# One loop over the steps of all tiles and both layers, with x split a tile ahead

## The chip, the core and the metric

The kernel runs on one core of a Trainium2 chip. The metric is the device time of one execution in microseconds (us); a lower time is better. Engines are named as in the profile: PE (TensorE), PEld (its weight loads), DVE (VectorE), ACT (ScalarE), POOL (GpSimd), SP (SyncE, which issues the transfers here).

## The reference

Attention without a softmax over keys, then two feed-forward layers on the same 2304 tokens of width 512:

```python
batch, n_heads, seq, head_dim = (4, 8, 576, 64)
# attention, per batch and head
q_s = exp(q - max(q, axis=-1));  q_s = q_s / (sum(q_s, axis=-1) + 1e-09)
k_s = exp(k - max(k, axis=2));   k_s = k_s / (sum(k_s, axis=2) + 1e-09)
kv = einsum('bhsd,bhse->bhde', k_s, v)
x = einsum('bhsd,bhde->bhse', q_s, kv)      # reshaped to (2304, 512)
# layer 1
h = x @ w_in                                 # (2304, 2048)
r = maximum(h, 0.0);  g = s * (r * r) + b
x = g @ w_out                                # (2304, 512)
# layer 2, other weights
h = x @ w_in
sp = log1p(exp(minimum(h, 20.0)))            # h itself where h > 20
g = h * tanh(sp)
out = g @ w_out
```

## The kernel before

Every fp32 product is made of three matmuls: each operand is split into a high part (a rounded copy, made by ACT) and a low part (the rest, made by DVE), and the products high*high, high*low and low*high are summed in one PSUM bank.

The tokens are cut into five tiles: tiles 0 to 3 have 512 tokens (`TILE`), tile 4 (`FULL`) has 256 (`LAST`). Layer 1 takes them in the order 0 to 4, layer 2 in the order 0, 4, 1, 2, 3 (`B_ORDER`). A tile has 16 steps (`FC`), one for each 128 columns of the 2048. A step of a tile is, on PE, `up` (12 matmuls into one of the H banks) and `down_a` or `down_b` (12 matmuls into the four Y banks, which sum over all 16 steps of a tile). `up` of a step runs `LAG_A` = 3 steps ahead of `down_a` in layer 1, and `LAG_B` = 4 steps ahead of `down_b` in layer 2, because ACT and DVE work on the step in between:

- layer 1: ACT `relu`, DVE `square`, ACT `g_hi`, DVE `g_lo`. `relu` of a step also waits until the slot of g that it writes has been used, that is for `down_a` of three steps before, which PE runs directly after the `up` of the same step. `up` uses two H banks (`HA`), and waits for the `relu` of two steps before.
- layer 2: ACT `exp_h`, DVE `min_e` and `m_of_e`, ACT twice in `rough_inverse`, DVE `rough_ratio`, `unity`, `ratio`, `gate`, ACT `g_hi_b`, DVE `g_lo_b`. DVE works on three steps at once. `up` uses four H banks (`HB`), and waits for the `gate` of four steps before.

Each tile ends with a drain: PE runs the last three or four `down` with no `up` between them. Meanwhile ACT and DVE split the next tile's x into `xs_hi` and `xs_lo` (`split_hi`, `split_lo`; the pair has one buffer, so the split waits for the last `up` of the tile), and then copy Y out of PSUM (`take_y`: banks 0 and 2 by ACT, 1 and 3 by DVE). Then the next tile begins with three or four `up` and no `down`.

The attention for the next batch is cut into four units (two heads each), which run inside the steps of layer 1 in the tiles 0 to 2, a unit every four steps: in the step that a unit starts DVE does `q_max`, `q_shift`, `k_max`, and at the end `q_sum`, `q_eps`, `q_inv`, `q_scale`; one step on `k_shift` (DVE) and `k_exp` (ACT); three steps on PE does `q_transpose` and `kv_product`, and DVE `kv_norm`; five steps on PE does `x_product` and DVE `take_x`. ACT copies the transposes out of PSUM (`take_qT`), and `kv_product`, which writes to the same bank, waits for that copy (`qT_taken`). The q of a unit is loaded when the q of the unit before has been transposed, its k and v when `kv_product` of the unit before is done. The weights are split inside the steps too: in tile 0 by the tables `FIRST_HI` (ACT) and `FIRST_LO` (DVE), in tile 4 by `NEXT_HI` and `NEXT_LO`, in the first tile of layer 2 by `LATE_PARTS`.

All engines work through their own instructions in the order of the program; only semaphores tie them together. Middle tiles are written once in a loop (`Fori`), the others in line.

Of the kernel before, what the change touches and what calls it, by code (L numbers as in the profile page):

```python
# [12 lines left out]
P = 128  # L13
# [9 lines left out]
def linear_attention_moe_kernel(nc, q, k, v, w_in1, w_out1, s, b, w_in2, w_out2, out):  # L23
# [27 lines left out]
    with ExitStack() as ctx:  # L51
# [153 lines left out]
        @block.sync
        def _(sp):
# [61 lines left out]
            with sp.Fori(0, NEXTRA - 1) as t:  # L268
                for p in range(1, NP):
                    load_unit(Unit(t + 1, p))  # L270
                load_unit(Unit(t + 2, 0))
            for p in range(1, NP):
                load_unit(Unit(NEXTRA, p))
# [55 lines left out]
        def _(act):  # L329
# [30 lines left out]
            def split_hi(T, src, x_units=None, parts=range(KC)):  # L360
                w = width(src)
                if not isinstance(T, int) or T > 0:
                    act.wait_ge(h_ready, FC * T)
                for i in parts:
                    if x_units is not None:
                        act.wait_ge(x_taken, 2 * (x_units + i + 1))
                    nc.scalar.activation(xs_hi[:, i, 0:w], xy_tile(i, src, w), ACT.Copy).then_inc(xhi_done, 1)

            def relu(T, f, w):
                c = FC * T + f  # L370
                act.wait_ge(h_ready, c + 1)
                if f >= LAG_A:
                    act.wait_ge(g_used, (FC - 1) * T + f - LAG_A + 1)
                nc.scalar.activation(g_raw[:, f % LAG_A, 1, 0:w], Hb[f % HA][:, 0:w], ACT.Relu).then_inc(ha_taken, 1)  # L374

            def g_hi(T, f, w):
                act.wait_ge(sq_done, FC * T + f + 1)
                nc.scalar.activation(g[:, f % LAG_A, 0, 0:w], g_raw[:, f % LAG_A, 1, 0:w], ACT.Identity,  # L378
                                     bias=b_col[:]).then_inc(ghi_done, 1)

            def take_y(T, src, w, banks, rows=False):
                for i in range(0, banks, 2):
                    act.wait_ge(y_ready, T + i + 1)
                    dst, y = (xy_tile(i, src, w), Y[i][:, 0:w]) if not rows else (
                        last_rows(i), Y[i].rearrange("p (a n) -> p a n", n=LAST))
                    nc.scalar.activation(dst, y, ACT.Copy).then_inc(y_taken_act, 1)
# [521 lines left out]
```

## Time and profile before

| | |
|---|---|
| median of 3 runs | 901.88 us (899.53 to 903.38) |
| the profiled execution's own time | 902.98 us |
| its span, first to last instruction | 901.2 us |
| mean granted TensorE clock | 0.981 of full speed; 0.50 from 503.0 to 506.4 and from 629.3 to 636.1 us |
| PE / DVE / ACT busy | 95% / 68% / 42% of the span |
| layer 2 begins | 488.2 us |
| bytes read and written | 36.15 MB, mean 40 GB/s |

"Busy" counts the time in which an engine executes; the ends of matmuls are modelled. A wait is idle time of an engine before an instruction, put down to the instruction whose end released it. Below, distances between the starts of neighbouring instructions are used where they run back to back, since that is what each costs its engine.

### The profile page before, as it was taken

What the parts mean: (1) busy time and instruction counts of PE and PEld (TensorE: products, weight loads), DVE (VectorE), ACT (ScalarE), POOL (GpSimd) and SP (SyncE); (2) the same over time, 40 slices, a digit from 0 to 9 for tenths busy, and PEclk for the clock granted to TensorE, in tenths of its full rate; (3) what the DMA queues carried; (4) which work ended last, traced back from release to release, by engine and by line L of the source; (5) the groups of instructions that cost most, each with busy time, mean ns of one, the idle gap of its engine ahead of it and who ended that gap; (6) DMA issues with size and microseconds to landing.
All of it is one profiled execution on the core that took longest, in us unless ns stands there. A gap on an engine that the chain in (4) does not pass through costs nothing.

```text
span 901.2 us, 11133 instructions
## 1 busy us (share of the span) xinstructions
PE 858.3 (95%) x4136; PEld 720.9 (80%) x4136; DVE 608.8 (68%) x1033; ACT 378.5 (42%) x621; POOL 30.5 (3%) x30
## 2 busy tenths in 40 slices
PE   2689999999999999999999899998999999999998
PEld 2568888888888888888998678897888788878886
DVE  5578875755576554322356889788697879777975
ACT  2245443423343333222356445455454445444543
POOL 2400000100000000000000000000000000000000
PEclk9599999999999999999999999999899999999999
DMA  8281111111101110000144000100000010000001
GB/s 204 76 290 40 40 40 40 40 40 40 40 13 39 39 27 1 1 0 1 47 158 171 0 1 1 47 1 1 24 0 1 1 47 0 0 10 37 0 0 47
DMA packets 60645, 36.15 MB, mean 40 GB/s; under 512 B 48320, under 2 KB 50368, under 8 KB 60608
## 3 DMA queue, kind: packets, MB, share of 16 engines
q1 hardware_dynamic: 60608, 35.66, 13.8%
q8 instruction: 23, 0.38, 0.2%
q14 instruction: 14, 0.11, 0.0%
HBM read 30.93 MB, written 4.72 MB: 40 GB/s over the span
## 4 chain that ended last, share of the span: by engine, by line
PE 80%; DVE 9%; ACT 5%; issue 4%; POOL 1%; DVEq 0%; ACTq 0%; POOLq 0%
PE H L790 38%; PE Y L804 20%; PE Y L818 16%; PE H L757 2%; PE H L778 1%; ACT t L452 1%; DVE g L696 1%; DVE t L668 1%; ACT t L454 1%; DVE wout_lo L592 1%; DVE t L673 1%; ACT wout_hi L353 1%; PE H L769 1%; DVE t L678 1%; DVE win_lo L592 1%
## 5 line engine op out<-in xcount | busy, mean ns | idle before, releaser
L790 PE MATMUL H<-xs_hi,win_hi 128*128 128x512 f32 (+1 forms) x640 | 240.4, 376 | 7.6 <-DVE g_raw L691 3.3
L790 PE MATMUL H<-xs_lo,win_hi 128*128 128x512 f32 (+1 forms) x640 | 236.7, 370 | 0.0
L790 PE MATMUL H<-xs_hi,win_lo 128*128 128x512 f32 (+1 forms) x640 | 236.6, 370 | 0.0
L818 PE MATMUL Y<-wout_hi,g 128*128 128x512 f32 x576 | 190.5, 394 | 5.5 <-DVE g L696 5.5
L804 PE MATMUL Y<-g,wout_hi 128*128 128x512 f32 (+1 forms) x640 | 183.2, 371 | 0.7 <-DVE g L576 0.7
L790 PEld LDWEIGHTS H<-xs_hi,win_hi 128*128 128x128 f32 x640 | 121.4, 190 | 30.0 <-DVE g_raw L691 4.0
L790 PEld LDWEIGHTS H<-xs_hi,win_lo 128*128 128x128 f32 x640 | 121.3, 190 | 20.6
L790 PEld LDWEIGHTS H<-xs_lo,win_hi 128*128 128x128 f32 x640 | 121.3, 190 | 20.5
L818 PEld LDWEIGHTS Y<-wout_hi,g 128*128 128x128 f32 x576 | 108.8, 189 | 31.1 <-DVE g L696 8.7
L804 PEld LDWEIGHTS Y<-g,wout_hi 128*128 128x128 f32 x640 | 115.2, 189 | 20.0 <-DVE g L576 0.9
L571 DVE SCALAR_TENSOR_TENSOR g_raw<-g_raw,s_col 128x512 f32<-128x512 f32 (+1 forms) x80 | 55.5, 694 | 95.9 <-ACT g_raw L374 95.6
L804 PE MATMUL Y<-g,wout_lo 128*128 128x512 f32 (+1 forms) x320 | 117.8, 368 | 0.0
L452 ACT ACTIVATE t<-t,two 128x512 f32<-128x512 f32 (+1 forms) x80 | 54.6, 682 | 142.1 <-DVE t L668 142.1
L374 ACT ACTIVATE g_raw<-H 128x512 f32<-128x512 f32 (+1 forms) x80 | 44.0, 550 | 165.1 <-PE Y L804 154.2
L818 PE MATMUL Y<-wout_lo,g 128*128 128x512 f32 x288 | 113.0, 392 | 0.0
L576 DVE SCALAR_TENSOR_TENSOR g<-g_raw,b_col,g 128x512 fp32r<-128x512 f32 (+1 forms) x80 | 55.9, 698 | 60.6 <-ACT g L378 60.6
L378 ACT ACTIVATE g<-g_raw,b_col 128x512 fp32r<-128x512 f32 (+1 forms) x80 | 54.2, 678 | 91.4 <-DVE g_raw L571 91.4
L804 PEld LDWEIGHTS Y<-g,wout_lo 128*128 128x128 f32 x320 | 60.3, 189 | 10.2
L818 PEld LDWEIGHTS Y<-wout_lo,g 128*128 128x128 f32 x288 | 54.5, 189 | 10.7
L673 DVE TENSOR_TENSOR t<-t,t 128x512 f32<-128x512 f32 (+1 forms) x80 | 51.1, 639 | 16.7 <-ACT t L454 8.9
L447 ACT ACTIVATE t<-H 128x512 f32<-128x512 f32 (+1 forms) x80 | 43.6, 544 | 39.2 <-PE H L790 39.2
L663 DVE TENSOR_SCALAR t<-t 128x512 f32<-128x512 f32 (+1 forms) x80 | 31.6, 395 | 34.4 <-ACT t L447 34.4
(71 smaller groups left out, 818.5 us busy)
## 6 DMA issues: line engine op xcount, KB each, us to landing
win_raw<-in_moe_w_in_dram SPq DMA_DIRECT2D x8, 1024.0 KB, 7.5
wout_raw<-in_moe_w_out_dram SPq DMA_DIRECT2D x8, 1024.0 KB, 5.1
g_flat<-in_v_dram SPq DMA_DIRECT2D x32, 144.0 KB, 3.3
out_dram<-xy SPq DMA_DIRECT2D x18, 256.0 KB, 2.1
qbuf<-in_q_dram SPq DMA_DIRECT2D x24, 144.0 KB, 2.9
kbuf<-in_k_dram SPq DMA_DIRECT2D x24, 144.0 KB, 3.1
raw<-in_q_dram SPq DMA_DIRECT2D x4, 288.0 KB, 4.6
raw<-in_k_dram SPq DMA_DIRECT2D x4, 288.0 KB, 7.7
```

The lines of the kernel that those rows point to most:

```text
L374: nc.scalar.activation(g_raw[:, f % LAG_A, 1, 0:w], Hb[f % HA][:, 0:w], ACT.Relu).then_inc(ha_taken, 1)
L378: nc.scalar.activation(g[:, f % LAG_A, 0, 0:w], g_raw[:, f % LAG_A, 1, 0:w], ACT.Identity, bias=b_col[:]).then_inc(ghi_done, 1)
L447: nc.scalar.activation(t1[:, f % 2, 0:w], Hb[f % HB][:, 0:w], ACT.Exp).then_inc(e_done, 1)
L452: nc.scalar.activation(t2[:, f % 2, 0:w], t1[:, f % 2, 0:w], ACT.Ln, bias=two[:]).then_inc(ln_done, 1)
L571: nc.vector.scalar_tensor_tensor(r, r, s_col[:], r, ALU.mult, ALU.mult).then_inc(sq_done, 1)
L576: nc.vector.scalar_tensor_tensor(g[:, f % LAG_A, 1, 0:w], g_raw[:, f % LAG_A, 1, 0:w], b_col[:], g[:, f % LAG_A, 0, 0:w].bitcast(F32), ALU ...
L592: nc.vector.tensor_tensor(lo, raw, hi.bitcast(F32), ALU.subtract).then_inc(win_ready if kind == 'in' else wout_ready, 1)
L663: nc.vector.tensor_scalar_min(t, t, EXP_CAP).then_inc(min_done, 1)
L673: nc.vector.tensor_tensor(t, t, t2[:, f % 2, 0:w], ALU.mult).then_inc(c_done, 1)
L790: last = nc.tensor.matmul(Hb[f % banks][:, 0:w], a[:, i, cols], m[:, i, 0:w], start=(i == 0 and n == 0), stop=(i == KC - 1 and n == XPASS ...
L804: last = nc.tensor.matmul(Y[i][:, 0:w], a[:, f, cols], g[:, f % LAG_A, m, 0:w], start=(f == 0 and n == 0), stop=(f == FC - 1 and n == XPAS ...
L818: last = nc.tensor.matmul(Y[i][:, :], g[:, f % LAG_B, a, rows], m[:, f, :], start=(f == 0 and n == 0), stop=(f == FC - 1 and n == XPASS - 1))
```

## The change

The steps of all tiles are numbered through (`c`, 16 a tile, 80 a layer), and all loops are written out. At the turn of a tile PE goes on alternating: the `up` of the next tile's first three (layer 2: four) steps stand between the last `down` of the tile. `take_y` of a tile moves into the next tile, to its step 2 in layer 1 (and in the first tile of layer 2), to its step 3 in the rest of layer 2; the first `down` of a tile now waits for all copies of the tile before. The high part of x has two buffers (`xhi0`, `xhi1`), its low part is written over x itself; a tile's x is split one piece at a time during the tile ahead, at the steps 5, 8, 11, 14 in layer 1, and 6, 8, 10, 12 in layer 2. The units of batch 1 now start at the steps 0, 3, 6, 9 of tile 0; those of the batches 2 and 3 at step 13 of the tile ahead and at the steps 1, 5, 9.

The diff, cut to its core:

```diff
+        def wait_used(engine, c):
+            if c % FC == FC - 1:
+                engine.wait_ge(y_ready, y_count(c // FC + 1))
+            else:
+                engine.wait_ge(g_used, (FC - 1) * (c // FC) + c % FC + 1)
+        START = {}
+        for batch in range(1, B):
+            for p in range(NP):
+                START[FC * (batch - 1) + (0, 3, 6, 9)[p] if batch == 1 else FC * (batch - 1) + (-3, 1, 5, 9)[p]] = (batch, p)
+        def unit_at(c):
+            return Unit(*START[c]) if c in START else None
+        def split_at(pos, f):
+            steps = (5, 8, 11, 14) if pos < TILES else (6, 8, 10, 12)
+            return steps.index(f) if pos + 1 < len(SRC) and f in steps else None
...
-            with act.Fori(1, NEXTRA) as t:
-                tile_a(t, True)
-                next_and_take_a(t, True)
+            for c in range(FC * TILES):
+                pos, f = c // FC, c % FC
+                relu(c, WIDTH[pos])
+                if unit_at(c - 2):
+                    take_qT(unit_at(c - 2))
+                g_hi(c, WIDTH[pos])
+                if pos > 0 and f == LAG_A - 1:
+                    take_y(pos - 1)
+                if unit_at(c):
+                    q_exp(unit_at(c))
+                if unit_at(c - 1):
+                    k_exp(unit_at(c - 1))
+                if pos == 0 and f in FIRST_HI:
+                    kind, i = FIRST_HI[f]
+                    hi_part(kind, 0, i)
...
+                if split_at(pos, f) is not None:
+                    split_hi(pos + 1, split_at(pos, f))
...
+            for c in range(FIRST, END):
+                pos, f = c // FC, c % FC
+                rough_inverse(c, WIDTH[pos])
+                if pos == TILES and f == LAG_A - 1 or pos > TILES and f == LAG_B - 1:
+                    take_y(pos - 1)
+                if c + 1 < END:
+                    exp_h(c + 1, WIDTH[(c + 1) // FC])
+                if c > FIRST:
+                    g_hi_b(c - 1, WIDTH[(c - 1) // FC])
...
-                split_lo(T + 1, nxt, range(KC - 1))
-                if attention:
-                    take_x(Unit(T + 1, NP - 1))
-                split_lo(T + 1, nxt, [KC - 1])
-                take_y(KC * T, T, w, KC)
...
+                if f == 0 and pos > 0:
+                    pe.wait_ge(y_taken_act, y_count(pos) // 2)
+                    pe.wait_ge(y_taken_dve, y_count(pos) // 2)
...
-                for f in range(FC + LAG_A):
...
+            for c in range(FIRST):
+                if unit_at(c - 5):
+                    x_product(unit_at(c - 5))
+                n = unit_at(c - 3)
+                if n and n.u > NP:
+                    q_transpose(n)
+                if c >= HA:
+                    pe.wait_ge(ha_taken, c - HA + 1)
+                up(c, HA)
+                if n and n.u == NP:
+                    q_transpose(n)
+                elif n:
+                    kv_product(n)
+                if c >= LAG_A:
+                    down_a(c - LAG_A)
```

How the order moves, at three places. First, ACT in tile 0, from `relu` of step 3 on. Before (L374 `relu`, L378 `g_hi`, L332 `q_exp`, L348 and L353 a high part of weights, L336 `k_exp`, L341 `take_qT`):

```order
L374 ACTIVATE g_raw<-H 128x512
L378 ACTIVATE g<-g_raw,b_col 128x512
L374 ACTIVATE g_raw<-H 128x512
L378 ACTIVATE g<-g_raw,b_col 128x512
L332 ACTIVATE qbuf<-qbuf 96x768
L348 ACTIVATE win_hi<-win_raw 128x4x512
L374 ACTIVATE g_raw<-H 128x512
L378 ACTIVATE g<-g_raw,b_col 128x512
L336 ACTIVATE kbuf<-kbuf 96x768
L374 ACTIVATE g_raw<-H 128x512
L341 ACTIVATE xy<-H 128x3x96 x2
```

The same stretch after (L396 `relu`, L400 `g_hi`, L353 `q_exp`, L357 `k_exp`, L369 the high part, L362 `take_qT`, L390 `split_hi`):

```order
L396 ACTIVATE g_raw<-H 128x512
L400 ACTIVATE g<-g_raw,b_col 128x512
L353 ACTIVATE qbuf<-qbuf 96x768
L396 ACTIVATE g_raw<-H 128x512
L400 ACTIVATE g<-g_raw,b_col 128x512
L357 ACTIVATE kbuf<-kbuf 96x768
L369 ACTIVATE win_hi<-win_raw 128x4x512
L396 ACTIVATE g_raw<-H 128x512
L362 ACTIVATE xy<-H 128x3x96 x2
L400 ACTIVATE g<-g_raw,b_col 128x512
L390 ACTIVATE xhi_60<-xy 128x512
```

The unit's `q_exp` and `k_exp` stand one step earlier, and its `take_qT` comes one `relu` after the high part of the weights, where two stood between them.

Second, DVE in the same stretch, from `g_lo` of step 2 on. Before (L544, L547, L551 `kv_norm`, L571 `square`, L576 `g_lo`, L592 a low part of weights, L510, L515, L505 the start of a unit):

```order
L576 SCALAR_TENSOR_TENSOR g<-g_raw,b_col,g 128x512
L544 TENSOR_SCALAR ksum<-H 64x1 x2
L547 RECIPROCAL kinv<-ksum 128x1
L551 TENSOR_SCALAR kv<-H,kinv 64x64 x2
L571 SCALAR_TENSOR_TENSOR g_raw<-g_raw,s_col 128x512
L576 SCALAR_TENSOR_TENSOR g<-g_raw,b_col,g 128x512
L592 TENSOR_TENSOR wout_lo<-wout_raw,wout_hi 128x2048
L510 TENSOR_REDUCE qmax<-qbuf 96x12
L515 TENSOR_TENSOR qbuf<-qbuf,qmax 96x2x6x64
L505 TENSOR_REDUCE kmax_68<-kbuf 96x128
```

After (L508, L513, L503 the start of a unit, L542, L545, L549 `kv_norm`, L567 `square`, L571 `g_lo`, L526, L531, L535, L517 its sum, reciprocal and scaling, L522 `k_shift`):

```order
L571 SCALAR_TENSOR_TENSOR g<-g_raw,b_col,g 128x512
L508 TENSOR_REDUCE qmax<-qbuf 96x12
L513 TENSOR_TENSOR qbuf<-qbuf,qmax 96x2x6x64
L503 TENSOR_REDUCE kmax_69<-kbuf 96x128
L542 TENSOR_SCALAR ksum<-H 64x1 x2
L545 RECIPROCAL kinv<-ksum 128x1
L549 TENSOR_SCALAR kv<-H,kinv 64x64 x2
L567 SCALAR_TENSOR_TENSOR g_raw<-g_raw,s_col 128x512
L571 SCALAR_TENSOR_TENSOR g<-g_raw,b_col,g 128x512
L592 TENSOR_TENSOR wout_lo<-wout_raw,wout_hi 128x2048
L526 TENSOR_REDUCE qsum<-qbuf 96x12
L531 TENSOR_SCALAR qeps<-qsum 96x12
```

The start of the second unit now stands ahead of `kv_norm` of the first and of `square` of the same step.

Third, DVE at the turn from tile 3 to tile 4 in layer 1. Before, all four pieces of the split and both copies of Y (L585) stand behind the last `g_lo` of the tile:

```order
L571 SCALAR_TENSOR_TENSOR g_raw<-g_raw,s_col 128x512
L576 SCALAR_TENSOR_TENSOR g<-g_raw,b_col,g 128x512
L564 TENSOR_TENSOR xs_lo<-xy,xs_hi 128x256 x4
L585 COPY xy<-Y 128x512 x2
```

After, the copies follow three steps of the new tile, whose rows have 256 elements:

```order
L567 SCALAR_TENSOR_TENSOR g_raw<-g_raw,s_col 128x256
L571 SCALAR_TENSOR_TENSOR g<-g_raw,b_col,g 128x256
L567 SCALAR_TENSOR_TENSOR g_raw<-g_raw,s_col 128x256
L571 SCALAR_TENSOR_TENSOR g<-g_raw,b_col,g 128x256
L567 SCALAR_TENSOR_TENSOR g_raw<-g_raw,s_col 128x256
L571 SCALAR_TENSOR_TENSOR g<-g_raw,b_col,g 128x256
L585 COPY xy<-Y 128x512 x2
```

The copies moved from the drain to behind `g_lo` of step 2, and the split is gone from the turn.

## Rows read from the trace of the kernel before

**Rows 1.** The page's first part, PE's share: busy us (share of the span) xinstructions.
```profile
PE 858.3 (95%) x4136; PEld 720.9 (80%) x4136; DVE 608.8 (68%) x1033; ACT 378.5 (42%) x621; POOL 30.5 (3%) x30
```

**Rows 2.** PE's waits over the span: us in total, times, longest.
```profile
PE Y L818 <- DVE g L696: 5.5, 7, 1.9
...
PE H L790 <- DVE g_raw L691: 3.3, 1, 3.3
PE H L790 <- ACT g_raw L374: 2.8, 1, 2.8
PE H L790 <- DVE xs_lo L564: 1.4, 2, 1.2
```

**Rows 3.** Busy time by stretch, with granted clock, at the layer-2 drain.
```profile
629.30:636.10 6.80, 6.27 (x15) 4.44 (x14) 2.63 (x6) 1.01 (x2) 0.00 (x0) 0.50 0.12 39
```

**Rows 4.** The chain that ended last, one `up` of layer 1: start, us.
```profile
410.10 2.72 PE H L790 x12
```

**Rows 5.** Timeline of ACT and DVE, that step: start, us, idle before.
```profile
410.20 0.60 ACT L374 ACTIVATE g_raw<-H 128x512 f32<-128x512 f32 x1 [3.30 <-PE Y L804]
411.62 0.72 ACT L378 ACTIVATE g<-g_raw,b_col 128x512 fp32r<-128x512 f32 x1 [0.82 <-DVE g_raw L571]
...
412.37 0.75 DVE L576 SCALAR_TENSOR_TENSOR g<-g_raw,b_col,g 128x512 fp32r<-128x512 f32 x1 [0.79 <-ACT g L378]
```

**Rows 6.** Groups of DVE from 64 to 440 us: copies of Y, mean ns.
```profile
L585 DVE COPY xy<-Y 128x512 f32 x4 | 2.8, 690 | 0.2
```

**Rows 7.** Timeline of DVE in tile 0, steps 3 to 5.
```profile
73.07 0.32 DVE L544 TENSOR_SCALAR ksum<-H 64x1 f32<-64x1 f32 x2
...
74.69 0.75 DVE L571 SCALAR_TENSOR_TENSOR g_raw<-g_raw,s_col 128x512 f32<-128x512 f32 x1 [0.48 <-ACT g_raw L374]
...
76.90 2.28 DVE L592 TENSOR_TENSOR wout_lo<-wout_raw,wout_hi 128x2048 fp32r<-128x2048 f32 x1
79.10 0.94 DVE L510 TENSOR_REDUCE qmax<-qbuf 96x12 f32<-96x768 f32 x1
...
82.39 0.74 DVE L571 SCALAR_TENSOR_TENSOR g_raw<-g_raw,s_col 128x512 f32<-128x512 f32 x1
...
84.66 0.95 DVE L528 TENSOR_REDUCE qsum<-qbuf 96x12 f32<-96x768 f32 x1
...
87.08 0.82 DVE L558 COPY xy<-H 128x288 f32<-128x288 f32 x2
87.83 0.94 DVE L524 TENSOR_TENSOR kbuf<-kbuf,kcol 96x768 f32<-96x768 f32 x1
88.69 0.74 DVE L571 SCALAR_TENSOR_TENSOR g_raw<-g_raw,s_col 128x512 f32<-128x512 f32 x1
```

**Rows 8.** Timeline of ACT in tile 0: a high part, and `take_qT`.
```profile
84.53 1.90 ACT L348 ACTIVATE win_hi<-win_raw 128x2048 fp32r<-128x2048 f32 x1
...
91.31 1.28 ACT L341 ACTIVATE xy<-H 128x288 f32<-128x288 f32 x2
```

**Rows 9.** Timeline of PE there: `kv_product` of the second unit.
```profile
92.69 0.57 PE L757 MATMUL H<-g_flat,kbuf 96*128 96x130 f32 x3
```

**Rows 10.** Transfers of k: KB each, median us from issue to landing.
```profile
kbuf<-in_k_dram SPq DMA_DIRECT2D x24, 144.0 KB, 3.1
```

**Rows 11.** Timeline of DVE in layer 2, 512 wide: two `gate`.
```profile
757.59 0.69 DVE L691 SCALAR_TENSOR_TENSOR g_raw<-g_raw,H 128x512 f32<-128x512 f32 x1
...
761.89 0.69 DVE L691 SCALAR_TENSOR_TENSOR g_raw<-g_raw,H 128x512 f32<-128x512 f32 x1
```

**Rows 12.** Timeline of DVE in layer 2, tile 4, 256 wide: two steps.
```profile
604.98 0.43 DVE L673 TENSOR_TENSOR t<-t,t 128x256 f32<-128x256 f32 x1 [0.24 <-ACT t L454]
...
607.63 0.43 DVE L673 TENSOR_TENSOR t<-t,t 128x256 f32<-128x256 f32 x1 [0.24 <-ACT t L454]
```

**Rows 13.** Timeline of PE in the same tile: two `down_b`.
```profile
604.56 0.40 PE L818 MATMUL Y<-wout_hi,g 128*128 128x512 f32 x1
...
607.38 0.40 PE L818 MATMUL Y<-wout_hi,g 128*128 128x512 f32 x1
```

More of the change, by code:

```diff
@@ L267, in _ @@
                 load_wout(0, i)
[L268 to L273, printed above, removed]
+            for u in range(NP + 1, B * NP):
+                load_unit(Unit(u // NP, u % NP))
             for i in range(NG):
@@ L381, in take_y, with split_hi @@
[L381 to L385, printed above, removed]
+            def split_hi(pos, i):
+                src, w = SRC[pos], WIDTH[pos]
+                if pos < TILES:
+                    act.wait_ge(x_taken, 2 * (NP * min(pos, B - 1) + i + 1))
+                else:
+                    act.wait_ge(y_taken_act, y_count(src + 1) // 2)
+                    act.wait_ge(y_taken_dve, y_count(src + 1) // 2)
+                if pos >= 2:
+                    act.wait_ge(h_ready, FC * (pos - 1))
+                nc.scalar.activation(xhi[pos % 2][:, i, 0:w], xy_tile(i, src, w), ACT.Copy).then_inc(xhi_done, 1)
@@ L654, in _ @@
-            tile_a(0, True)
-            with dve.Fori(1, NEXTRA) as t:
-                tile_a(t, True)
-            for T in (FULL - 1, FULL):
-                tile_a(T, False)
-            def min_e(T, f, w):
-                dve.wait_ge(e_done, FC * T + f + 1)
-                t = t1[:, f % 2, 0:w]
+            for c in range(FC * TILES):
+                pos, f = c // FC, c % FC
+                w = WIDTH[pos]
+                if unit_at(c):
+                    q_max(unit_at(c))
+                    q_shift(unit_at(c))
+                    k_max(unit_at(c))
+                if unit_at(c - 5):
+                    take_x(unit_at(c - 5))
+                if unit_at(c - 1):
+                    k_shift(unit_at(c - 1))
+                if unit_at(c - 3):
+                    kv_norm(unit_at(c - 3))
+                square(c, w)
+                g_lo(c, w)
+                if pos > 0 and f == LAG_A - 1:
+                    take_y(pos - 1)
+                if pos == 0 and f in FIRST_LO:
+                    kind, part = FIRST_LO[f]
+                    lo_part(kind, 0, part)
+                if pos == FULL and f in NEXT_LO:
+                    kind, part = NEXT_LO[f]
+                    lo_part(kind, 1, part)
+                if unit_at(c):
+                    q_sum(unit_at(c))
+                    q_eps(unit_at(c))
+                    q_inv(unit_at(c))
+                    q_scale(unit_at(c))
+                if split_at(pos, f) is not None:
+                    split_lo(pos + 1, split_at(pos, f))
@@ L749, in _ @@
+            take_y(len(SRC) - 1)
         @block.tensor
```

460 lines of the change are left out of this document (181 added, 279 removed).

## The prediction

> **What bounds the kernel now.** I read the page's first part, then the waits of PE, then the timelines of ACT and DVE around each place that the change touches. PE is busy for 858.3 of 901.2 us [rows 1], and its matmuls are the same before and after, so the change can only give back PE's idle time and its time at half clock. Its waits are short [rows 2]. The wait of 2.8 us (for a `relu`, at 60.6 us) is at the very start of tile 0 and stays. There is no other wait in layer 1 worth naming until the end of tile 4: the drains of tiles 0 to 3 cost nothing, since three `down_a` (8.2 us) cover the split and three `up` (8.2 us) cover the copies of Y. What is left is the turn into layer 2 and the first steps there (waits of 3.3 and 1.2 us, and part of the 5.5 and 1.4), the end of layer 2's tile 4, and 0.4 us at each of the last two turns. Each such wait costs some 0.17 us more than the row says, because the end of a matmul is modelled (0.39 us long, 0.23 us from start to start). To that come the stretches at half clock: 6.8 us at the end of layer 2's tile 4 [rows 3] and 3.4 us at 503 us (the table above), which cost half their length, 5.1 us. The ceiling of the gain is 5.5 + 3.3 + 1.4 + 0.7 (a small wait for `g_lo`) + 1.6 + 5.1 = 17.6 us.
>
> **The turns of layer 1.** I count from T, the end of the last `down_a` of a tile, which in the new order comes in step 2 of the next tile. PE then does one `up`, 2.72 us [rows 4], and arrives at the first `down_a` of the new tile, which waits for all four copies of Y. But both copying engines have `relu`, `square`, `g_hi` and `g_lo` of step 2 ahead of the copies, and that `relu` waits for the same `down_a`, as every `relu` of layer 1 does. In a plain step with T at 410.10, `relu` starts at 410.20 and DVE's `g_lo` ends at 413.12 [rows 5], 3.0 us after T. Two copies of 0.69 us on DVE [rows 6] end 4.35 us after T. PE waits 4.35 - 2.72 = 1.65 us. Into tile 4 the `up` is half as long (1.4 us) while the copies stay 512 wide and the chain before them shrinks by about 0.9 us: I take 2.05. Into tiles 1 and 2 `k_shift` of a unit stands ahead of `square` and adds 0.1 to 0.4: I take 1.9 each. Four turns: 1.9 + 1.9 + 1.65 + 2.05 = 7.5 us lost, where now nothing is. Below: 4 us, if only the part behind `g_hi` counts (ACT's own copies end at 3.3 us). Above: 10 us, if DVE comes late from the units. The split, taken out of the turn, gives nothing back: it was hidden.
>
> **Tile 0.** The units of batch 1 now follow each other every three steps. A step's DVE work, from start to start [rows 7]: the start of a unit 82.39 - 79.10 = 3.3 us, `kv_norm` 74.69 - 0.48 - 73.07 = 1.1, `square` with `g_lo` 84.66 - 82.39 = 2.3, a low part 79.10 - 76.90 = 2.2, the q part 87.08 - 84.66 = 2.4, `k_shift` 88.69 - 87.83 = 0.9. With the second unit at step 3, DVE is free for it at 73.07. Its k lands 3.1 us [rows 10] after the first unit's `kv_product`, near 75.2, which costs 0.3. Then: start 3.3, `kv_norm` 1.1, so `square` of step 3 comes at 77.8 instead of 74.69; with `g_lo` 2.3, the low part 2.2 and the q part 2.4, q is scaled at 84.7. PE wants to transpose it at step 6. In the trace `kv_product` of step 7 starts at 92.69 [rows 9], behind 0.45 us of transposes, an `up` of 2.72 [rows 4] and a gap of 0.2, so step 7 begins at 89.3, and step 6 one step of 5.44 earlier, at 83.9; it slips by 0.1: 0.7 us of wait. Then `k_shift` to 85.6, `square` of step 4, ACT's `g_hi` to 87.0, `k_exp` (0.75) to 87.8, the high part of weights that stands in step 4 (1.9 [rows 8]) to 89.6, `relu` to 90.1, and `take_qT` (1.3 [rows 8]) to 91.3. PE has done its transposes (0.45) and the `up` of step 6 (2.72) at 87.9, and `kv_product` waits for `take_qT`: 3.3 us. Today this wait is just avoided: `take_qT` ends at 92.6 and `kv_product` starts at 92.69 [rows 8, 9], a step later in PE's program. The change pulls PE's part forward by a step and ACT's hardly at all. The third unit has no high part in the step ahead of its `take_qT` (`FIRST_HI` has 4 and 10, not 7), and I get no wait. The fourth has: the same count gives 0.3 + 3.3 us. An `x_product` waits 0.4. Sum 0.7 + 3.3 + 0.3 + 3.3 + 0.4 = 8.0, less the 0.7 of small gaps that are there now and fall into these: 7.3, of which I take 7.0. Below: 0, if the transfer and the order ahead leave DVE earlier. Above: 11, if k lands later and both places slip by 2. Nothing is gained in return: the x of tile 1 was ready in time anyway.
>
> **The turn into layer 2.** PE waits there for DVE, which does one step in 761.89 - 757.59 = 4.3 us [rows 11], and in the steps 0, 3 and 6 more than double that, with a low part and the wait for ACT's high part. So what counts is when DVE begins. The first `up` of layer 2 no longer stands behind the drain and the split, but DVE still has the last two steps of tile 4, a low part (2.2), and now four pieces of the split among the narrow steps before. I get its first `min_e` 3.0 us earlier. From that go two narrow copies of Y (0.7) and a narrow piece of split (0.4): 2.0 us gained, visible at the `down_b` of step 5. Waits earlier than that one are only moved. Below: 0. Above: 9.5, all of the waits and the half clock there.
>
> **Tile 4 in layer 2.** Here DVE takes 607.63 - 604.98 = 2.65 us a step [rows 12] and PE 607.38 - 604.56 = 2.82 [rows 13], so DVE regains 0.17 us a step. The change puts into this tile two copies of 0.69 and four pieces of the 512-wide split of the next tile. DVE's piece waits for ACT's piece, which stands behind `exp_h` and `g_hi_b`: about 1.7 us each instead of 0.7, an estimate from the two ACT operations ahead. That is 1.4 + 6.8 = 8.2 us more on an engine with 2.7 us to spare in 16 steps, and a lead of about 4 us over PE. My count: PE waits 1.5 us at step 4 for the copies (DVE still behind from the tile before), 2.1 us in the steps 9 to 11, 2.7 us at step 4 of the next tile, 6.3 in all. The drain there costs now 3.0 us of waits, 0.9 of modelled ends and 3.4 of half clock [rows 2, 3]: 7.3. Gain 1.0. Below a loss of 3, above a gain of 7.
>
> **The last two turns.** With DVE abreast of PE the copies end about 5.75 us after the `up` of step 3, and PE needs them after 5.44: 0.3 us each against 0.6 now. Gain 0.5. Ends, store and start stay.
>
> **Sum.** 901.2 + 7.5 + 7.0 - 2.0 - 1.0 - 0.5 = 912.2 us of span; 1.8 us lie around it in the profiled execution (902.98), which is 1.1 above the median of the runs shown: 914.0 - 1.1 = 912.9 us.
>
> **The rivals.**
> - *The clock falls with the new waits.* Before the 6.8 us at half clock [rows 3] PE had idled three times, at most 1.9 us; the wait of 2.8 us [rows 2] was followed by none. The two waits of 3.3 us in tile 0 and the 2.7 us in layer 2 could each bring 3.4 to 6.8 us at half clock, 1.7 to 3.4 us: some 5 us, 918. The Trainium skill (TensorE: Matmul & The Clock Gate, Part 1) has the slow clock as the default, which idling brings back; rows 3 agree, with 0.50 in that stretch.
> - *Only the turns cost.* If `take_qT` in tile 0 ends before PE's 87.9, which takes 3.4 us less on the chain of five instructions that I added, 7 us fall away: 905.9, no difference that counts.
> - *The other side: the drains were the cost.* If DVE carries pieces and copies in its idle time (it is busy for 68% [rows 1]), all waits of layer 2 go, and the copies end before PE's `down_a`. It decides at the turn of layer 1: copies within 2.72 us of T. Price: 901.9 - 10 to 17.6, about 888. Against it: `relu` waits for T itself.
> - *The loops cost.* Taken branches could stall engines, and the change has none. In the chain that ended last, the matmuls of layer 1's loop follow each other over its turn without a gap, so a gain above 1 us has no row. The Trainium skill (Runtime: NRT & Kernel Launch, Instruction fetch mechanics) says that a taken branch to a page of code that isn't loaded stalls; by it every turn would show a gap, and this trace has none.
>
> **How the numbers follow.** My own count 0.53, with 904 to 919 for itself (its terms at half of their bounds); clock 0.13; only the turns 0.15; the other side 0.13; loops 0.03; no effect at all 0.03. A difference of 0.5%, 4.5 us, is about what a measurement of this kernel can tell from none. Faster 0.16, the same 0.18, slower 0.66. The range goes from 900, which takes in "only the turns" and half of the near cases, to 919, with the clock: about 0.18 is left out, mostly below.
>
> **What the profile after would show.** Right, if the waits of PE name the copies of Y (L585, or ACT's) four times in layer 1 with 1.6 to 2.1 us each, and `take_qT` twice in tile 0 with about 3 us, and if `down_b` still waits for `g_lo_b` in the first and second tile of layer 2. The first is wrong if PE runs through the turns; the second if `kv_product` has no wait before 140 us. The sum is wrong above all if DVE's backlog in layer 2's tile 4 is not what I count, or if the clock falls.

## The result, and the profile after

The changed kernel takes 924.12 us (median of 4 runs, 922.13 to 927.08); the kernel before, run beside it, 901.92 (899.53 to 903.38). The ratio is 1.0254, with a 95% interval from 1.0231 to 1.0276: slower, as forecast, but by 22 us where 11 were forecast, and outside the range given. The profiled execution took 925.83 us, with a span of 924.0 and a mean clock of 0.976.

The page's first part and the waits of PE over the span answer to [rows 1, 2]:

```profile
PE 866.1 (94%) x4136; PEld 725.5 (79%) x4136; DVE 607.1 (66%) x1033; ACT 377.1 (41%) x621; POOL 28.3 (3%) x30
```

```profile
PE H L736 <- DVE xy L556: 10.3, 3, 4.2
PE Y L776 <- DVE xy L585: 6.9, 4, 2.0
PE Y L795 <- DVE xy L585: 5.4, 3, 2.8
...
PE H L760 <- ACT g_raw L396: 2.9, 1, 2.9
PE Y L795 <- DVE g L686: 1.9, 3, 1.1
PE H L760 <- DVE xlo L561: 1.6, 1, 1.6
PE H L745 <- DVE kv L549: 1.1, 1, 1.1
PE H L760 <- DVE g_raw L682: 0.7, 1, 0.7
```

The second row is the four turns that were forecast. The first was not in the prediction's sum: L736 is `q_transpose`, and it waits for L556, `take_x` of the unit before. The third, fifth, sixth and eighth belong to the turn into layer 2 and to layer 2. PE's busy time grew by 7.8 us with the same matmuls, and some 5 of that is the clock: after the prologue, the stretches at half clock in the trace start at 64.1, 91.4, 115.3, 139.2, 531.7 and 671.7 us, 3.4 us each, 20.5 us against 10.2 before. Four of the six lie in tile 0, where there was none; the first of them, at 64.1 us, follows a wait that was there before as well (`relu`, 2.8 us then and 2.9 us now). Two of them as windows (length; busy time and instructions of PE, PEld, DVE, ACT, POOL; clock; DMA share; GB/s), to be held against [rows 3]:

```profile
91.40:94.80 3.40, 3.40 (x9) 2.67 (x9) 2.49 (x3) 2.15 (x5) 0.00 (x0) 0.50 0.38 87
...
671.70:675.10 3.40, 3.40 (x9) 2.64 (x8) 3.24 (x6) 1.35 (x2) 0.00 (x0) 0.50 0.46 154
```

**A turn of layer 1**, the timeline where tile 1 ends:

```profile
284.97 0.60 ACT L396 ACTIVATE g_raw<-H 128x512 f32<-128x512 f32 x1 [3.56 <-PE Y L776]
...
287.15 0.75 DVE L571 SCALAR_TENSOR_TENSOR g<-g_raw,b_col,g 128x512 fp32r<-128x512 f32 x1 [0.80 <-ACT g L400]
287.82 1.28 DVE L585 COPY xy<-Y 128x512 f32<-128x512 f32 x2
...
289.25 0.70 PE L776 MATMUL Y<-g,wout_hi 128*128 128x512 f32 x2 [1.66 <-DVE xy L585]
```

It is [rows 5, 6] in a line: `relu` starts as the last `down_a` ends, `g_lo` is done 2.9 us after the start of `relu`, then two copies, and the `down_a` that wanted them 1.7 us before they were there.

**Tile 0**, the timeline of DVE, PE and ACT around the start of the second unit's work on PE, beside [rows 7 to 9]:

```profile
76.72 1.53 DVE L503 TENSOR_REDUCE kmax<-kbuf 96x128 f32<-96x768 f32 x1 [1.95 <-DMA kbuf<-in_k_dram]
...
79.36 1.24 PE L745 MATMUL H<-xy,kv 128*128 128x288 f32 x4 [1.13 <-DVE kv L549]
...
85.19 0.95 DVE L517 TENSOR_TENSOR qbuf<-qbuf,qinv 96x768 f32<-96x768 f32 x1
86.06 0.95 DVE L522 TENSOR_TENSOR kbuf<-kbuf,kcol 96x768 f32<-96x768 f32 x1
86.93 0.74 DVE L567 SCALAR_TENSOR_TENSOR g_raw<-g_raw,s_col 128x512 f32<-128x512 f32 x1
...
88.47 0.75 DVE L571 SCALAR_TENSOR_TENSOR g<-g_raw,b_col,g 128x512 fp32r<-128x512 f32 x1 [0.79 <-ACT g L400]
89.25 0.82 DVE L556 COPY xy<-H 128x288 f32<-128x288 f32 x2
...
90.22 0.69 PE L736 MATMUL H<-ident,qbuf 96*128 96x96 f32 x6 [4.17 <-DVE xy L556]
...
91.35 1.21 ACT L362 ACTIVATE xy<-H 128x288 f32<-128x288 f32 x2
```

The first unit's x stood ready in PSUM from 80.2 us (`x_product` at 79.36). DVE copies it only at 89.25, at the head of its own step 5, behind all of its step 4. The second unit's q is scaled by 86.06, which is when PE gets there. But its transposes write to the same two banks, so they wait until the copy is done at 90.1. Before, the units were four steps apart: the copy ran at 87.08 [rows 7] and was done 1.3 us before PE came to the transposes, in the timeline of the kernel before:

```profile
89.21 0.66 PE L769 MATMUL H<-ident,qbuf 96*128 96x96 f32 x6
```

All three units after the first now pay: 4.2, 3.2 and 3.0 us.

**Layer 2**, the third tile's step 4 in the timeline:

```profile
669.88 0.68 DVE L585 COPY xy<-Y 128x512 f32<-128x512 f32 x1
...
670.71 0.47 PE L795 MATMUL Y<-wout_hi,g 128*128 128x512 f32 x1 [2.80 <-DVE xy L585]
```

DVE runs without a gap for more than 9 us ahead of that copy; it is simply behind.

### The profile page after: what moved, and what is told of

Read it like the earlier page. It is cut to its first block, busy times and chain, and to the rows that moved or that the text cites. A ratio compares the mean times of both kernels' runs of the same rounds, so it can differ in the third digit from the quotient of the medians.

```text
span 924.0 us, 10489 instructions
## 1 busy us (share of the span) xinstructions
PE 866.1 (94%) x4136; PEld 725.5 (79%) x4136; DVE 607.1 (66%) x1033; ACT 377.1 (41%) x621; POOL 28.3 (3%) x30
## 4 chain that ended last, share of the span: by engine, by line
PE 69%; DVE 16%; ACT 7%; issue 5%; POOL 1%; DMA 1%; SPq 0%; POOLq 0%; ACTq 0%
PE H L760 31%; PE Y L776 17%; PE Y L795 16%; ACT t L462 2%; PE H L724 2%; DVE g L686 2%; DVE t L663 2%; DVE t L658 2%; DVE wout_lo L592 1%; ACT g L400 1%; DVE g_raw L567 1%; PE H L745 1%; DVE win_lo L592 1%; ACT t L464 1%; DMA kbuf<-in_k_dram 1%
## 5 line engine op out<-in xcount | busy, mean ns | idle before, releaser
L760 PE MATMUL H<-xhi,win_hi 128*128 128x512 f32 (+1 forms) x640 | 242.9, 380 | 5.3 <-ACT g_raw L396 2.9
L760 PE MATMUL H<-xhi,win_lo 128*128 128x512 f32 (+1 forms) x640 | 238.5, 373 | 0.0
L760 PE MATMUL H<-xlo,win_hi 128*128 128x512 f32 (+1 forms) x640 | 238.1, 372 | 0.0
L795 PE MATMUL Y<-wout_hi,g 128*128 128x512 f32 x576 | 192.8, 395 | 7.5 <-DVE xy L585 5.4
L760 PEld LDWEIGHTS H<-xhi,win_hi 128*128 128x128 f32 x640 | 122.5, 191 | 28.5 <-ACT g_raw L396 3.3
L760 PEld LDWEIGHTS H<-xlo,win_hi 128*128 128x128 f32 x640 | 122.4, 191 | 21.1
L760 PEld LDWEIGHTS H<-xhi,win_lo 128*128 128x128 f32 x640 | 122.1, 191 | 21.1
L567 DVE SCALAR_TENSOR_TENSOR g_raw<-g_raw,s_col 128x512 f32<-128x512 f32 (+1 forms) x80 | 55.6, 695 | 121.9 <-ACT g_raw L396 121.6
L396 ACT ACTIVATE g_raw<-H 128x512 f32<-128x512 f32 (+1 forms) x80 | 44.1, 551 | 206.0 <-PE Y L776 206.0
L571 DVE SCALAR_TENSOR_TENSOR g<-g_raw,b_col,g 128x512 fp32r<-128x512 f32 (+1 forms) x80 | 55.9, 698 | 61.7 <-ACT g L400 61.7
L400 ACT ACTIVATE g<-g_raw,b_col 128x512 fp32r<-128x512 f32 (+1 forms) x80 | 54.3, 678 | 89.0 <-DVE g_raw L567 89.0
L682 DVE SCALAR_TENSOR_TENSOR g_raw<-g_raw,H 128x512 f32<-128x512 f32 (+1 forms) x80 | 50.7, 634 | 2.8
```

The lines of the kernel that those rows point to most:

```text
L396: nc.scalar.activation(g_raw[:, slot(c), 1, 0:w], Hb[c % HA][:, 0:w], ACT.Relu).then_inc(ha_taken, 1)
L400: nc.scalar.activation(g[:, slot(c), 0, 0:w], g_raw[:, slot(c), 1, 0:w], ACT.Identity, bias=b_col[:]).then_inc(ghi_done, 1)
L567: nc.vector.scalar_tensor_tensor(r, r, s_col[:], r, ALU.mult, ALU.mult).then_inc(sq_done, 1)
L571: nc.vector.scalar_tensor_tensor(g[:, slot(c), 1, 0:w], g_raw[:, slot(c), 1, 0:w], b_col[:], g[:, slot(c), 0, 0:w].bitcast(F32), ALU.add, ...
L682: nc.vector.scalar_tensor_tensor(t3, t3, -1.0, Hb[c % HB][:, 0:w], ALU.mult, ALU.mult).then_inc(hb_taken, 1)
L760: last = nc.tensor.matmul(Hb[c % banks][:, 0:w], a[:, i, cols], m, start=(i == 0 and n == 0), stop=(i == KC - 1 and n == XPASS - 1))
```

## The experiments

Every kernel ran beside the kernel before on the chip that it ran on. That kernel's median was 901.92 us for the changed kernel, 901.39 for e1 to e4, 901.13 for e5 to e8 and 900.12 for e9 to e11, so a difference between two medians from different groups is uncertain by up to 1.8 us; the ratios take this out.

**Two suspected causes one by one.** e1: `take_x` of batch 1 one step earlier.

```diff
+                if unit_at(c - 4) and unit_at(c - 4).b == 1:
+                    take_x(unit_at(c - 4))
                 if unit_at(c):
...
-                if unit_at(c - 5):
+                if unit_at(c - 5) and unit_at(c - 5).b > 1:
                     take_x(unit_at(c - 5))
```

> The changed kernel, but DVE does take_x of the units of batch 1 one step earlier, ahead of k_shift, square and g_lo of the fourth step instead of behind them. Theory: in tile 0 PE's transposes wait (4.2, 3.2 and 3.1 us, 10.3 in all) for take_x of the unit before, and DVE reaches it 3.2 to 5.4 us later than it could. Expected: the first wait falls to about 1.5, the others to under 1, 7 to 8 us saved, and with them two or three stretches at half clock of 3.4 us (1.7 us each): 911 to 915 against 924. Rival, as in the prediction: DVE and ACT are late as a whole, so the wait only moves on to kv_product, which waits for take_qT behind the high part of weights, about 3 us in two places: then 918 to 921.

920.01 us (919.13 to 920.61), ratio 1.0208 [1.0187, 1.0228]. The transposes' wait fell from 10.3 to 1.1 us, and most of it came back one place on. Waits and timeline of e1:

```profile
PE H L726 <- issue: 5.8, 2, 2.9
```

```profile
86.68 1.89 ACT L369 ACTIVATE win_hi<-win_raw 128x2048 fp32r<-128x2048 f32 x1
...
88.95 1.17 ACT L362 ACTIVATE xy<-H 128x288 f32<-128x288 f32 x2
...
90.22 1.99 PE L726 MATMUL H<-g_flat,kbuf 96*128 96x130 f32 x11 [2.88 <-issue]
```

L726 is `kv_product`. Its row names no releaser, but it starts as ACT's `take_qT` (L362) ends, and that stands behind the high part (L369): the wait that the prediction had named, there in the second and the fourth unit. It had been hidden by a longer one on the same path. The rival holds, in the time too.

e2: the copies of Y first in the turns of layer 1.

```diff
+                if pos > 0 and f == LAG_A - 1:
+                    take_y(pos - 1)
                 relu(c, WIDTH[pos])
...
                 g_hi(c, WIDTH[pos])
-                if pos > 0 and f == LAG_A - 1:
-                    take_y(pos - 1)
```

and the same on DVE ahead of `square`.

> The changed kernel, but in layer 1 the copies of Y stand ahead of relu (ACT) and square (DVE) in step 2 of a tile instead of behind g_hi and g_lo. Theory: PE waits 1.8 to 2.1 us at each of the four turns because the copies stand behind the chain of four operations that starts at the same moment. Copied first they end 1.4 us after T, and PE needs them 2.7 us after T (1.4 into the narrow tile): no wait at three turns, under 0.3 at the fourth, 7.3 to 7.6 us saved, 916 to 917. Rival: the chain of step 2, now 1.3 us later, is itself what PE waits for next, and less than 3 us are saved, 921 or more.

915.35 us (912.72 to 917.76), ratio 1.0144 [1.0119, 1.0169]: 8.8 us less than the changed kernel. The timeline of e2 at the same turn:

```profile
282.20 1.28 DVE L585 COPY xy<-Y 128x512 f32<-128x512 f32 x2
...
284.16 0.62 PE L776 MATMUL Y<-g,wout_hi 128*128 128x512 f32 x2
```

All four waits are gone, and no other took their place in layer 1.

e3: k isn't loaded for the units after the first of batch 1 (their k is what lies in the buffer), so that DVE's `k_max` waits for no transfer; `k_shift` waits for `kv_product` of the unit before instead. It leaves out a part of the work, and its values are not the kernel's.

```diff
                 load_q(n)
-                load_k(n)
                 load_v(n)
...
-                dve.wait_ge(n.k_in, n.n_in)
+                dve.wait_ge(n.k_in, n.n_in if n.first else 32)
...
                 dve.wait_ge(kcol_done, n.u + 1)
+                if n.u > NP:
+                    dve.wait_ge(kv_done, n.u)
```

> The changed kernel without the loads of k for the units after the first of batch 1 (they work on what is in the buffer, so the values are others; k_shift waits for kv_product of the unit before in place of the load). It asks how much of tile 0's wait is the transfer: DVE waits there 2.0, 2.4 and 3.4 us for k, which is loaded only when PE is through with the k before. If the transfer is half of the cause, take_x comes that much earlier, and PE's transposes wait about 2.2, 0.8 and 0 instead of 4.2, 3.2 and 3.1: 7 us less and two stretches at half clock less, 913 to 917. If DVE's work between is the cause alone, the time that the transfer leaves is used up by waits for relu, and under 3 us are saved: 921 or more.

914.16 us (912.54 to 917.85), ratio 1.0154 [1.0125, 1.0183], 10 us less. The waits of PE in e3:

```profile
PE H L737 <- DVE xy L557: 5.6, 2, 4.2
```

The second unit still waits 4.2 us, the third no more, the fourth 1.5; 2.2, 0.8 and 0 were expected, so the time came out as forecast and the places did not. The transfer isn't what makes the second unit late; DVE's waits for it (1.95, 2.4 and 3.4 us, growing from unit to unit) are what keeps the third late, and the fourth for a good part. Not all of the 10 us is shown to be the transfer's: in tile 0 PE waits 5.8 us less than in the changed kernel (the `x_product` included), and 6.8 us are at half clock in place of 13.6. Of that difference one stretch, 3.4 us, is the one at 64.1 us.

e4: e1 and e2 together, and the copies first in layer 2 too (ahead of `rough_inverse` on ACT, ahead of `ratio` on DVE).

> The changed kernel with take_x early in batch 1 and with the copies of Y ahead of the chain at all turns, of layer 2 too (ACT: ahead of rough_inverse; DVE: ahead of ratio and gate). If the costs add up: 924 less 7.5 and 4 in tile 0, less 7.5 at the turns of layer 1, less 3 to 5 in layer 2 (PE waits there 5.4 us for the copies in three places): 900 to 903, the time before. If in layer 2 the backlog of DVE is the cause and the place of the copies is not, 903 to 906.

906.95 us (905.22 to 909.00), ratio 1.0061 [1.0036, 1.0085]. It missed the 900 to 903, and the rival's 906, mainly in tile 0, where `kv_product` still waits 5.7 us. In layer 2 PE's waits hardly fell, they moved: those for the copies from 5.4 to 2.1 us, while those for `g_lo_b` rose from 1.9 to 4.5. From the last `down_a` of layer 1 to the last `down_b` PE takes 394.5 us; in e3, whose layer 2 is that of the changed kernel and, like e4's, has no half clock, it takes 397.4. So there the copies in front are worth 2.9 us. The waits of PE in e4:

```profile
PE H L726 <- issue: 5.7, 2, 2.9
...
PE Y L797 <- DVE g L688: 4.5, 4, 1.6
...
PE Y L797 <- DVE xy L585: 2.1, 2, 1.4
```

**The place behind it.** e5 is e4 with two of ACT's high parts moved.

```diff
-        FIRST_HI = {2: ('out', 1), 4: ('in', 2), 6: ('out', 2), 8: ('in', 3), 10: ('out', 3)}
-        FIRST_LO = {1: ('in', 1), 3: ('out', 1), 5: ('in', 2), 7: ('out', 2), 9: ('in', 3), 11: ('out', 3)}
+        FIRST_HI = {2: ('out', 1), 5: ('in', 2), 6: ('out', 2), 8: ('in', 3), 11: ('out', 3)}
+        FIRST_LO = {1: ('in', 1), 3: ('out', 1), 6: ('in', 2), 7: ('out', 2), 9: ('in', 3), 12: ('out', 3)}
```

> The kernel with all three reorderings, and in tile 0 the high parts of steps 4 and 10 (and the low parts that follow them) one step later, so that none stands on ACT in the step ahead of a unit's take_qT. Theory (kv_product waits 2.9 us twice, for take_qT, which stands behind the high part): these two waits go, and with them the half clock that follows: 907 less 5.7 less 0 to 3.4, 898 to 902. Rival (take_qT is late because the transposes and relu are late, not because of the high part): the waits stay and the time stays at 905 to 908.

903.15 us (901.03 to 905.48, 10 runs), ratio 1.0025 [1.0012, 1.0038], 3.8 us less than e4, where 5 to 9 were expected. The waits of PE in e5:

```profile
PE H L762 <- ACT g_raw L396: 4.8, 2, 2.9
...
PE H L726 <- issue: 2.5, 3, 1.1
```

`kv_product` waits 2.5 us instead of 5.7, but besides the first wait of tile 0 (2.9 us) an `up` now waits 1.9 us for a `relu` that stands behind the high part of step 6. The high part was the cause of more than half of that wait. Of the two orders tried at three steps a unit, neither is free; others were not tried.

e6: the changed kernel with one distance of four steps. In tile 0 the fourth piece of the split is put at step 15, ahead of `relu` and `square`.

```diff
-... FC * (batch - 1) + (0, 3, 6, 9)[p] if batch == 1 ...
+... FC * (batch - 1) + (0, 4, 7, 10)[p] if batch == 1 ...
-            steps = (5, 8, 11, 14) if pos < TILES else (6, 8, 10, 12)
+            steps = (5, 9, 12, 15) if pos == 0 else (5, 8, 11, 14) if pos < TILES else (6, 8, 10, 12)
```

> The changed kernel with the units of batch 1 at the steps 0, 4, 7, 10 instead of 0, 3, 6, 9: one of the three distances is four steps as before the change, the other two stay three; the pieces of the split follow at 5, 9, 12, 15. Theory (at a distance of three steps the transposes have to wait for take_x of the unit before, and for the start of their own unit on DVE): the first of the three waits of the transposes, 4.2 us, goes, the other two of about 3 stay; with the half clock after it 924 less 4.2 less 0 to 1.7, 918 to 920. Rival (the waits come from DVE being overfull in tile 0 whatever the distance): all three stay in some form, 922 to 925.

918.73 us (914.52 to 921.99), ratio 1.0180 [1.0148, 1.0212]. The waits of PE in e6:

```profile
PE H L740 <- DVE xy L558: 7.0, 3, 3.8
```

In its trace the second unit's transposes start without a wait, the other two wait 3.8 and 2.7 us (the third wait of the row, 0.5 us, is the first unit of batch 2). The time is within the 918 to 920 expected. At four steps the wait goes and at three it stays: the distance is the cause.

e7: none of the work is moved, but PE works through the waits.

```diff
+                if c >= HA:
+                    pe.wait_ge(ha_taken, c - HA + 1)
+                if n and n.b == 1 and n.u > NP:
+                    for _ in range(12):
+                        nc.tensor.matmul(Hb[c % HA][:], win_hi[:, 0, 0:P], win_hi[:, 0, 0:TILE], start=True, stop=True)
                 if n and n.u > NP:
                     q_transpose(n)
-                if c >= HA:
-                    pe.wait_ge(ha_taken, c - HA + 1)
```

The wait for the H bank moves ahead, because the added matmuls write to it.

> The changed kernel with 12 more matmuls of 512 columns (2.7 us, results unused) on PE ahead of the transposes of the second, third and fourth unit of batch 1, where PE now stands idle for 3.0 to 4.2 us. The waits themselves stay filled, not shortened. Theory (the half clock in tile 0 comes from PE standing idle there): the three stretches at 0.50 between 85 and 145 us, 3.4 us each, go, and the time falls by up to 5.1 us, to 919 to 921. Rival (the clock falls at these places for another reason, or at random): the stretches stay and the time is 924 to 926.

920.38 us (918.10 to 923.44), ratio 1.0214 [1.0180, 1.0247], 3.7 us less with 36 matmuls more. The same stretch of tile 0 as a window, first of the changed kernel, then of e7:

```profile
84.00:145.00 61.00, 50.70 (x230) 41.34 (x229) 42.71 (x61) 24.64 (x33) 1.41 (x2) 0.92 0.15 35
```

```profile
84.00:145.00 61.00, 59.40 (x289) 49.02 (x288) 44.75 (x67) 26.05 (x35) 1.41 (x2) 1.00 0.19 44
```

The clock stays at 1.00, so at these three places it falls because PE stands idle there, and a wait of 3 us costs up to 1.7 us more than it lasts. The Trainium skill (TensorE: Matmul & The Clock Gate, Part 1) says that idling brings the slow clock back; these two rows agree.

**Layer 2.** e8 is e5, with DVE's pieces one step after ACT's, and the pieces for layer 2's first tile at other steps of tile 4.

```diff
+        LATE_LO = {f + 1: part for f, part in LATE_PARTS.items()}
...
-                if pos == TILES and f in LATE_PARTS:
-                    kind, i = LATE_PARTS[f]
+                if pos == TILES and f in LATE_LO:
+                    kind, i = LATE_LO[f]
                     lo_part(kind, 1, i)
-                if c < END and split_at(pos, f) is not None:
-                    split_lo(pos + 1, split_at(pos, f))
+                if c < END and f and split_at(pos, f - 1) is not None:
+                    split_lo(pos + 1, split_at(pos, f - 1))
...
-            steps = (5, 8, 11, 14) if pos < TILES else (6, 8, 10, 12)
+            steps = (5, 8, 11, 14) if pos < FULL else (6, 8, 10, 12)
```

> As e5, and in layer 2 DVE's low parts of weights and its pieces of the split one step later than ACT's high ones, so that DVE doesn't stand idle for ACT; the pieces of x for layer 2's first tile at the steps 6, 8, 10, 12 of tile 4. Theory (the rest of layer 2's waits, some 8 us, comes from DVE standing behind ACT's pieces): 2 to 6 us less than e5, 894 to 899, with fewer waits of down_b for g_lo_b and of up for the low piece. Rival (DVE's own work is what is too long there): within 1.5 us of e5.

893.74 us (891.91 to 898.05), ratio 0.9917 [0.9898, 0.9936], 9.4 us less than e5 on the same chip: more than the 2 to 6 of the theory. The waits of DVE for ACT's high piece of x, first in e5, then in e8:

```profile
DVE xlo L561 <- ACT xhi L390: 32.4, 20, 2.9
```

```profile
DVE xlo L562 <- ACT xhi L391: 7.5, 6, 1.8
```

e11 makes the same edit alone, in the changed kernel.

> The changed kernel with one edit: in layer 2 DVE's low parts of weights and low pieces of x one step after ACT's high ones, and the pieces for layer 2's first tile at the steps 6, 8, 10, 12. Layer 1 stays with its turns and its tile 0. Theory (DVE's idle time behind ACT's pieces is what feeds layer 2's waits, as between e5 and e8): layer 2's waits fall from 10 to some 3 us, 924 less 5 to 9, 915 to 919. Rival (the gain between e5 and e8 hung on the copies of Y standing first in layer 2): the wait for the copies stays, 920 to 924.

912.19 us (911.38 to 918.99), ratio 1.0152 [1.0125, 1.0179]. That is 11.9 us less than the changed kernel by the medians and 0.0102, or 9.2 us, by the ratios. By the traces layer 2 is 9.0 us shorter than in the changed kernel, and 7.5 shorter than in e3, which has the same layer 2 as the changed kernel and, like e11, no half clock there; so 7.5 us belong to the edit and the rest of the 9.0 to the clock. The waits for the copies fell from 5.4 to 3.5 us, those for `g_lo_b` are gone, and that for the low piece fell from 1.6 to 0.2: the theory holds, with more than it had, and the rival only for a part. The waits of e11 in layer 2:

```profile
PE Y L796 <- DVE xy L586: 3.5, 2, 2.4
...
PE H L761 <- DVE xlo L562: 0.2, 1, 0.2
```

The edit has two halves, DVE's pieces one step later and other steps for the pieces of layer 2's first tile. They were not run apart.

**A better kernel.** e9 is e8 with e6's distances, and the parts of weights where no `take_qT` follows.

```diff
-        FIRST_HI = {2: ('out', 1), 5: ('in', 2), 6: ('out', 2), 8: ('in', 3), 11: ('out', 3)}
-        FIRST_LO = {1: ('in', 1), 3: ('out', 1), 6: ('in', 2), 7: ('out', 2), 9: ('in', 3), 12: ('out', 3)}
+        FIRST_HI = {2: ('out', 1), 4: ('in', 2), 6: ('out', 2), 7: ('in', 3), 10: ('out', 3)}
+        FIRST_LO = {1: ('in', 1), 3: ('out', 1), 5: ('in', 2), 8: ('out', 2), 9: ('in', 3), 12: ('out', 3)}
```

> As e8, with the units of batch 1 at the steps 0, 4, 7, 10, the split of tile 1's pieces at 5, 9, 12, 15, and the parts of the weights where no take_qT follows. Theory (what is left in tile 0, some 6 us of waits and 3 to 10 us at half clock, comes from three units at a distance of three steps): the first of the waits and up to 2 us of the second go, 2 to 5 us less than e8's 893.7, 889 to 892. Rival (DVE and ACT are full in tile 0 at any of these orders): 893 to 895.

886.84 us (886.20 to 890.88), ratio 0.9861 [0.9841, 0.9881]: 1.4% faster than the kernel before. That is 6.9 us less than e8 by the medians and 5.0 by the ratios, at or beyond the upper end of the 2 to 5 expected: the theory holds. These are its page's PE row and all waits of PE after the prologue:

```profile
PE 852.4 (96%) x4136; PEld 718.1 (81%) x4136; DVE 607.7 (69%) x1033; ACT 381.3 (43%) x621; POOL 29.4 (3%) x30
```

```profile
PE H L767 <- ACT g_raw L397: 3.2, 2, 2.8
PE H L731 <- issue: 1.1, 3, 0.5
PE Y L802 <- DVE xy L588: 0.9, 1, 0.9
...
PE H L767 <- DVE xlo L564: 0.2, 1, 0.2
```

e10 is e9 with `B_ORDER = (0, 1, 2, 3, FULL)`.

> As e9, with layer 2's tiles in the order 0, 1, 2, 3, 4, so that the 256-wide tile comes last instead of second. Theory (in the narrow tile DVE has 0.17 us to spare in a step and pays for 512-wide pieces and copies; as last tile it has only narrow work, and its end holds a shorter chain, copy and store): 1 to 3 us less than e9, about 888. Rival (after the low parts come a step later nothing waits there any more, and at the end DVE's lead is lost in the narrow tile): the same as e9 within 1 us, or slower by up to 2.

889.58 us (888.72 to 890.74), ratio 0.9887 [0.9871, 0.9903], 2.7 us slower than e9 by the medians, 2.3 by the ratios: the theory fails, and the rival is right in direction. Its waits are those of e9, so the narrow tile needs no relief any more. The profiled executions differ by 1.9 us (887.0 and 885.1 of span): 0.8 of it lies ahead of the first `up` of layer 1, which the edit doesn't touch, 0.6 in layer 2 and 0.5 behind the last `down_b`. So at most 1.1 us of these 1.9 can be the order's.

## Why the prediction was wrong

**The turns of layer 1: right.** Forecast 7.5 us; the trace has 6.9 of waits, with the modelled ends 7.6, and e2 gives 8.8 back by the medians.

**Tile 0: the step that failed.** The prediction took 7.0 us here, and said that `kv_product` would wait for `take_qT` in the second and fourth unit and that the third would not wait. Measured: waits of 10.3 and 1.1 us and ends of 0.7, less the 0.7 of gaps that were there, 11.4 us; and four stretches at half clock, 6.8 us. That makes 18.2, 11.2 more than the term. The sum was made of spans, and on spans it missed by 924.0 - 912.2 = 11.8 us: these 11.2, 0.1 at the turns and 0.8 in layer 2 (below), less 0.3 ahead of and behind the two layers. Of the 18.2 us, 1.7 are the stretch at 64.1 us, which 7 of the 13 profiles lack (last section); the median of the runs is 1.7 us below the profiled one. Three things went wrong in the term:

- The chain was followed along the unit's own data (q scaled at 84.7, measured 86.06; `take_qT` done at 91.3, measured 92.6) and not along the banks. `q_transpose` also waits for `take_x` of the unit before, and three steps are too few for that. For the second unit the number came out all the same, by luck: forecast 0.7 + 3.3, measured 4.2, but at another instruction and for another reason. The forecast wait lay underneath, as e1 shows (1.1 + 2.9 us). The third unit has no high part ahead but has the same banks: forecast 0, measured 3.2.
- k was to cost 0.3 us each in the second and the fourth unit. DVE waits 1.95, 2.4 and 3.4 us for it. It lands 4.2, 4.5 and 4.4 us after `kv_product` of the unit before, where 3.1 were counted, and DVE comes to `k_max` 2.2, 2.1 and 0.9 us after that `kv_product`: PE, held up by its waits, frees the buffer ever later against DVE. With `kv_norm` behind it in DVE's order, that makes the first `x_product` late too (1.1). Without the load (e3) the kernel takes 10 us less, 5.8 of them as waits of PE in tile 0.
- The clock. The rival "the clock falls with the new waits" was right in its mechanism, as e7 shows, but stood outside the sum with 0.13. Three of the four stretches in tile 0 follow the new waits; at 1.7 us each they make 5.1 us, about what the rival had priced.

**Layer 2: right in sum.** Forecast 3.5 us gained. From the last `down_a` of layer 1 to the last `down_b` PE takes 410.7 us before, and 398.9 after, to which belong the three `up` of layer 2 that now stand ahead of the first mark, 8.2 us: 407.1, 3.6 us gained, 1.7 of it clock. Ahead of the first mark `up` now waits 1.6 us for the low piece, where `down_a` waited 0.7 for `g_lo`; with that 0.9 us the gain is 2.7. The waits in the narrow tile's part of the count were forecast at 1.5, 2.1 and 2.7 us and are 0.5, 1.5 and 2.8. The last place is step 4 of the third tile, as forecast. DVE's piece does wait for ACT's: ahead of the four pieces in the narrow tile DVE stands idle for 1.55, 1.33, 1.34 and 1.33 us, so a piece costs about 2.0 us where the forecast had 1.7. e8 and e11 show that this was the largest cost in layer 2, and that it goes with their edit.

**The other rivals.** "Only the turns cost" falls with the 10.3 us. "The drains were the cost" falls for this kernel (`relu` does wait for T), but the time that it gave can be had: apart from the first wait of tile 0, e9 has no wait over 1 us left, and takes 13.3 us less than the kernel before beside it, where the rival had 10 to 17.6. "The loops cost" would leave layer 1 shorter wherever no wait is added, and tile 1 shows nothing of it: from the last `down_a` of tile 0 to its own last one PE takes 98.7 us before, in the loop, and 98.7 in e2, written out. The loop cost nothing there; whether its code ever had to be fetched anew no run shows. In the rival on the clock one reading was off: of the three waits named ahead of the 6.8 us at half clock, the third (0.5 us at 631.3) lies inside that stretch.

## What to carry to other kernels

When units of work that share a buffer are moved closer together, follow the buffer as well as the data: ask when its last reader, in the order of that reader's engine, lets go of it. Behind the wait that a trace names there may be a second one nearly as long, so one removal can give little, and the whole set has to go before it pays. An engine that works in order should get a piece that depends on another engine one step after it was made, and what PE waits for next should stand first in the step, ahead of work with time to spare. That was worth 8.8 us at the four turns of layer 1, and 2.9 us in layer 2, where DVE was behind as a whole.

## What the runs showed of the hardware

- Idle time of the same length is followed by half clock (0.50, the lower of the two levels) in one execution and not in another. Every kernel has the first wait of tile 0 (2.8 to 2.9 us, near 60 us). Half clock follows it in the profiles of the changed kernel, e1, e2, e4, e6 and e8, and doesn't in those of before, e3, e5, e7, e9, e10 and e11. The wait of 2.0 us at the turn into tile 4 is followed by 3.4 us at 0.50 in e1, e6 and e7, and not in the changed kernel, e3 and e11. The Trainium skill (TensorE: Matmul & The Clock Gate, Part 1) calls the rise of the clock at the start of a kernel run-variable. These traces agree, with the stretch at 0.50 that ends before tile 0: it is 17.1 us long in e1 and 23.9 us in the changed kernel. That is about the rise; the rows above show the same of the fall.
- That goes with a spread between executions. The first `up` of layer 1 starts at 51.55 us in the changed kernel's profile and at 48.48 in e1's, with the same program up to there, so a part of the difference between two profiles is no work of the edit. The four runs of the changed kernel reach from 922.13 us at a mean clock of 0.981 to 927.08 at 0.978, with 925.83 at 0.976 for the profiled one; e9's profile has no half clock after the prologue.
